# A third pair of query buffers, other places for some work of ScalarE and VectorE, and an end flag made and read earlier, in a fused attention and mixture-of-experts kernel

## The chip, the core and the metric

The kernel runs on one core of a Trainium2 chip. The metric is device time in microseconds, from start to end of one launch; lower is better. The kernel before was run three times: 861.81, 862.79 and 864.39 us, median 862.79 us.

## The reference, cut to what matters

Attention with a squared ReLU instead of a softmax, for 8 batches of 3072 rows, and then a mixture of 8 experts with one expert for each token and room for 768 tokens in each expert:

```python
scores = scale * np.matmul(z, z.transpose(0, 2, 1))     # z: 8 x 3072 x 64
attn = np.maximum(scores, 0.0) ** 2
x = (u * np.matmul(attn, v)).reshape(B * S, D)          # u, v: 8 x 3072 x 256
expert_idx = np.argmax(x @ w_gate, axis=1)              # 8 experts, capacity 768
for i in range(N):                                      # in order of the tokens
    e = expert_idx[i]
    if counts[e] < capacity:
        disp[e, counts[e]] = x[i]; counts[e] += 1       # kept, in the next free row
h = np.maximum(np.einsum('ecd,edf->ecf', disp, w1), 0.0)
y = np.einsum('ecf,efd->ecd', h, w2)
out[i] = gate_w[i] * y[expert_idx[i], pos[i]]           # only for kept tokens
```

Once all eight experts are full, no later token has an effect, so the attention of later rows need not be computed.

## The kernel before

**Stages.** The attention runs in groups n of 384 query rows (3 tiles of 128), 8 groups for each batch. With these inputs it runs groups 0 to 17 whole and the first part of group 18; then a flag says that every expert is full. The experts follow (from 605.87 us on in the profile), 16 blocks of 384 rows, each through w1 and w2.

**A group.** A group has 12 doubles c = 0 to 11, each of two chunks of 128 keys. TensorE (PE) makes scores in bursts of four doubles (`burst`, `scores`, the matmuls of L725): at c = 0 the scores of doubles 3 to 6, at c = 4 those of 7 to 10, at c = 8 those of double 11 and of doubles 0 to 2 of the next group. ScalarE (ACT) does the ReLU (`do_relu`, L533) and the square (`do_square`, L537) of each double, VectorE (DVE) splits the result into a high and a low half (`do_hi`, L1052, `do_lo`, L1058), and PE weighs v with it (`weigh`, 18 matmuls for a double, L760 to L764). ACT runs three doubles ahead of PE: in its step c it squares double c + 3 and relus double c + 4. A burst waits until the scores before it have been read (`relu_done`). Values go in high and low halves through three matmuls each, to keep precision.

**Queries and keys.** The group loop is a runtime loop, so the queries of a group are copied to fixed buffers, in two copies with the halves of partitions exchanged: `q_now` for the scores of the group itself and `q_next` for the first three doubles of the next group. GpSimd (POOL) issues these copies in `queries`, at the end of its body for group n, behind the three indirect DMAs that scatter the rows of group n - 1 to the experts (L446), the reading of the flag, the wait for these scatters to land (`scattered`, after which it frees the row buffer, `row_free`) and the wait for the burst at c = 8. PE waits for `loaded_q_now` at c = 0.

**The rows of the group before.** While PE weighs group n, the other engines route the rows of group n - 1. DVE takes them out of PSUM (`gate_x`, L1101 and L1105, at the end of its step c = 11 of group n - 1), ACT takes sums of their absolute values (L559) and high halves (L564), DVE the low halves (L1199), SyncE's queue (SP) transposes them with three DMAs (L303, `xT`), and PE multiplies with `w_gate` (L842, logits) inside double 3, behind a wait for `loaded_xT`. DVE finds each row's expert (`route_rows`, at its c = 3), PE counts (`counts_of_tiles`, L781 and L784, behind the burst at c = 4), and DVE makes positions, slots and the flag `full` (L1152 to L1172). PE's matmuls of double 4, tile 2, wait for `counts_read`.

**The flag.** `both_parts` gives each engine's body two parts with `load_end` between them: wait for `flag_ready`, load `full` into the register that ends the loop, skip the second part if it is zero. With `END_AT` = 5, PE, ACT, SP and POOL read it with double 5 done, DVE one step before. At the end, PE waits for the drains of ACT (L639) and DVE (L1357), `attention_over`, before its first matmul of the experts.

**Work for the next batch and the experts** has fixed places in the steps. In groups 1, 2, 9, 10 and 17 ACT takes four sums of |v| (`v_sum`, L508), one in each of its steps 6, 7, 8 and 9 (`SUM_AT`), each followed by a wait for its own semaphore. In groups 3 and 11 the norms of z are taken and DVE makes new scales in its steps 8 to 10. In group 8 ACT makes the high halves of the first expert's weights (`split_w_hi`, L636) in steps 7, 8 and 10, and DVE takes the maxima of the second expert's weights (`w_max`, L1323) in groups 8 to 11 (`W_MAX1_IN`). At the start of groups 0, 8 and 16 SP loads the next batch's z and v (L317, L322).

**Group 0** is written out by hand (`peeled`). In it the last quarter of the keys is made by ACT with two copies (`z_hi`, L520) in its step 1, behind the ReLU of double 5, and by DVE (L1010, L1017). PE needs those keys, and the ReLU of double 6, for its burst at c = 4.

## Time and profile before

| | kernel before |
|---|---|
| three runs, median | 861.81, 862.79, 864.39; 862.79 us |
| the profiled execution | 863.23 us, of which the span from the first to the last instruction is 861.4 us |
| PE busy with matmuls | 834.5 us (97% of the span) |
| PE weight loads (beside the matmuls) | 667.3 us (77%) |
| DVE busy | 630.0 us (73%) |
| ACT busy | 567.0 us (66%) |
| POOL busy | 170.4 us (20%) |
| mean granted TensorE clock | 0.996 |

Read it so: the span is the part that the instructions fill, and 1.8 us of the profiled execution lie around it. A PE that is busy 97% of the span leaves 26.9 us in which it does nothing, and a time at half clock counts as busy. The list of waits says what PE waited for; the chain of work that ended last, in order of time, gives the starts of PE's bursts, from which a group's length can be read; the timelines of ACT and DVE show how far ahead of PE they are.

### The profile page before, as it was taken

The numbers are of one execution on the slowest core, as the hardware profiler recorded it, in microseconds if no ns is written. First come the engines' busy times: TensorE is split into PE (matmuls) and PEld (weight loads), VectorE is DVE, ScalarE is ACT, GpSimd is POOL, SyncE is SP. The second block draws the span as 40 slices with busy tenths as digits, with TensorE's granted clock in tenths as the row PEclk, the third lists the DMA queues.
The fourth block names the chain that finished last, engine by engine and source line by source line (L and its number), as shares of the span: only waits on it lengthen the run. The fifth ranks groups of instructions, "written<-read, shape, count | busy, mean of one in ns | idle before, by whom it ended". The sixth has DMA issues, their size and how long they took to land.

```text
span 861.4 us, 25760 instructions
## 1 busy us (share of the span) xinstructions
PE 834.5 (97%) x8414; PEld 667.3 (77%) x8414; DVE 630.0 (73%) x1354; ACT 567.0 (66%) x866; POOL 170.4 (20%) x204
## 2 busy tenths in 40 slices
PE   6899999999999979999999999999999999999997
PEld 5778778788888868778788888887777777777776
DVE  7886877889989858887888888777554655565521
ACT  7877776778877758776878787678534434435422
POOL 3002112112221203202302311210121221211212
PEclk9999999999999989999999999999999999999999
DMA  7923244264334733233324425722616325415101
GB/s 290 377 80 113 55 156 179 59 187 166 118 86 128 264 88 110 84 99 110 120 78 131 139 60 156 284 61 73 156 44 167 115 68 159 143 46 152 55 18 37
DMA packets 109399, 107.90 MB, mean 125 GB/s; under 512 B 68749, under 2 KB 95578, under 8 KB 108352
## 3 DMA queue, kind: packets, MB, share of 16 engines
q1 hardware_dynamic: 100640, 87.29, 33.0%
q0 software_dynamic: 8736, 20.31, 6.7%
q8 instruction: 14, 0.23, 0.1%
q14 instruction: 9, 0.07, 0.0%
HBM read 40.03 MB, written 44.93 MB: 99 GB/s over the span
## 4 chain that ended last, share of the span: by engine, by line
PE 72%; issue 6%; DVE 6%; ACT 6%; DMA 5%; SPq 3%; DVEq 1%; ACTq 1%; POOL 0%; POOLq 0%
PE Sc L893 15%; PE O L760 11%; PE Sc L725 11%; PE O L764 10%; PE O L762 10%; PE O L916 3%; PE O L918 3%; PE O L920 3%; DMA xT<-xrow 2%; SPq L303 2%; DVE attn_hi L1052 2%; PE Sc L918 2%; PE Sc L916 2%; PE Sc L920 2%; ACT attn L533 2%
## 5 line engine op out<-in xcount | busy, mean ns | idle before, releaser
L760 PE MATMUL O<-vS,attn_hi 128*128 128x256 f16 x1332 | 363.4, 273 | 1.7 <-DVE vS L1036 1.7
L762 PE MATMUL O<-vS,attn_hi 128*128 128x256 f16 x1332 | 363.1, 273 | 0.0
L764 PE MATMUL O<-vS,attn_lo 128*128 128x256 f16 x1332 | 363.0, 273 | 0.0
L533 ACT ACTIVATE attn<-Sc 128x768 f32<-128x768 f32 x226 | 179.6, 795 | 61.5 <-PE Sc L725 58.3
L1058 DVE TENSOR_TENSOR attn_lo<-attn,attn_hi 128x768 f16<-128x768 f32 x224 | 214.4, 957 | 6.5
L537 ACT ACTIVATE attn<-attn 128x768 f32<-128x768 f32 x225 | 189.5, 842 | 10.1 <-ACT xT L508 2.9
L1052 DVE CAST attn_hi<-attn 128x768 f16<-128x768 f32 x224 | 125.0, 558 | 58.2 <-ACT attn L537 48.1
L760 PEld LDWEIGHTS O<-vS,attn_hi 128*128 128x128 f16 x1332 | 130.1, 98 | 29.3 <-issue 11.7
L764 PEld LDWEIGHTS O<-vS,attn_lo 128*128 128x128 f16 x1332 | 130.3, 98 | 15.2
L762 PEld LDWEIGHTS O<-vS,attn_hi 128*128 128x128 f16 x1332 | 130.3, 98 | 14.2
L1368 DVE SCALAR_TENSOR_TENSOR rawv<-Sc,rawv 128x768 f16<-128x768 f32 x63 | 60.2, 956 | 110.5 <-ACT rawv L646 61.2
L446 POOL DMA_INDIRECT disp<-xrow,slot x54 | 64.6, 1196 | 361.3 <-DVE slot L1171 350.4
L646 ACT ACTIVATE rawv<-Sc 128x768 f16<-128x768 f32 x63 | 51.0, 810 | 100.9 <-PE Sc L893 99.7
L725 PE MATMUL Sc<-q_now,zP 64*128 64x128 f16 (+1 forms) x801 | 90.4, 263 | 5.2 <-DMA q_now<-zQ 4.6
L725 PE MATMUL Sc<-q_now,zQ 64*128 64x128 f16 (+1 forms) x801 | 89.9, 263 | 0.0
L893 PE MATMUL Sc<-vS,w1h 128*128 128x384 f16 x384 | 78.1, 326 | 0.0
L725 PEld LDWEIGHTS Sc<-q_now,zP 64*128 64x128 f16 x801 | 55.3, 95 | 25.6 <-issue 16.1
L916 PE MATMUL O<-w2s,rawv 128*128 128x256 f16 x256 | 69.8, 273 | 0.0
L920 PE MATMUL O<-w2s,rawv 128*128 128x256 f16 x256 | 69.8, 273 | 0.0
L918 PE MATMUL O<-w2s,rawv 128*128 128x256 f16 x256 | 69.8, 273 | 0.0
L485 POOL DMA_INDIRECT out<-attn,vS x48 | 47.0, 979 | 114.0 <-ACT attn L658 100.8
L725 PEld LDWEIGHTS Sc<-q_now,zQ 64*128 64x128 f16 x801 | 55.1, 95 | 6.9
(167 smaller groups left out, 1025.0 us busy)
## 6 DMA issues: line engine op xcount, KB each, us to landing
out<-empty SPq DMA_DIRECT2D x16, 1536.0 KB, 5.9
wraw<-in_moe_w SPq DMA_DIRECT2D x16, 1024.0 KB
rawv<-in_v SPq DMA_DIRECT2D x14, 768.0 KB, 7.9
ubuf<-in_u SPq DMA_DIRECT2D x19, 384.0 KB, 3.2
disp<-vS SPq DMA_DIRECT2D x8, 774.0 KB, 11.5
rawz<-in_z SPq DMA_DIRECT2D x3, 768.0 KB
q_now<-zP POOLq DMA_DIRECT2D x18, 96.0 KB, 4.2
q_now<-zQ POOLq DMA_DIRECT2D x18, 96.0 KB, 4.2
```

The costliest lines, as they stand in the source:

```text
L533: act.activation(attn_place(c), score_place(c), ACT.Relu).then_inc(s["relu_done"], 1)
L537: act.activation(attn[:, c % BUFS, :, :], attn[:, c % BUFS, :, :], ACT.Square, scale=ROOT_C).then_inc(s["square_done"], 1)
L725: ins = nc.tensor.matmul(to, keys[r], queries[r][:, columns], start=at == 0, stop=at == len(terms) - 1)
L760: nc.tensor.matmul(o_part(t), hi, v[:, 0:D], start=c == 0 and j == 0 and t % 2 == 0, stop=False, skip_group_check=True)
L762: nc.tensor.matmul(o_part(t), hi, v[:, D:2 * D], start=False, stop=False, skip_group_check=True)
L764: ins = nc.tensor.matmul(o_part(t), lo, v[:, 0:D], start=False, stop=c == PAIRS - 1 and j == 1, skip_group_check=True)
L893: ins = nc.tensor.matmul(Sp[:, 2 * (p % 2) + fi, 0:GROUP], w[par][:, m, f * P:(f + 1) * P], xt[k][:, x + m, :], start=(at == 0), stop=(at ...
L916: nc.tensor.matmul(y_part(t), hi, w2s[:, par, f, 0:D], start=f == 0, stop=False, skip_group_check=True)
L918: nc.tensor.matmul(y_part(t), hi, w2s[:, par, f, D:2 * D], start=False, stop=False, skip_group_check=True)
L920: ins = nc.tensor.matmul(y_part(t), lo, w2s[:, par, f, 0:D], start=False, stop=f == FC - 1, skip_group_check=True)
L1052: dve.tensor_copy(attn_hi[:, b, :, :].rearrange("p j n -> p (j n)"), attn[:, b, :, :].rearrange("p j n -> p (j n)")).then_inc(s["hi_done"], 1)
L1058: dve.tensor_tensor(attn_lo[:, b, :, :], attn[:, b, :, :], attn_hi[:, b, :, :], ALU.subtract).then_inc(s["lo_done"], 1)
```

## The change

- A third pair of query buffers, `q_last`. Double 11's scores take their queries from it and no longer from `q_now`, so `q_now` is free after the burst at c = 4. POOL issues the copy to `q_now` for the next group as the first thing of its second part, after a wait for that burst and ahead of the wait for `scattered` and of `row_free`. The copies to `q_last` and `q_next` are issued where those to `q_now` and `q_next` were; PE waits for `q_last` at c = 8.
- ACT's four sums of |v| stand together in its step 7 (`SUMS_AT`), and so do the four conversions of the first expert's weights in group 8 (`W_HI_IN`). DVE's four maxima of the second expert's weights are all in its step 8.
- In group 0, ACT's two copies for the last keys go to steps 0 and 1, ahead of the ReLU of double 3 and of the square of double 4; DVE's part of them goes ahead of its v conversion. The scaling of `w_gate` goes from DVE's steps 8 and 10 to steps 5 and 7.
- The flag: DVE keeps, from step to step, how many rows each expert still lacks (`need`, times 1024, and zero when no group follows). When the counts arrive, one instruction subtracts them (`lack`) and a maximum over the experts, with a zero beside them, is the flag. Before, the flag took a sum, a subtraction, a minimum and a comparison, between steps of the routing. `END_AT` is 4: the flag is read with double 4 done (DVE: with its step 3 done), and if it is zero the group ends there. The test itself is the same: it goes on while an expert lacks rows.

The diff, without declarations of buffers:

```diff
             queries(q_now, 1, "loaded_q_now")
+            queries(q_last, 1, "loaded_q_last")
             queries(q_next, 2, "loaded_q_next")
...
                 def rest():
+                    wait_apart(pool, s["scores_ready"], n * PAIRS + PAIRS - 1)
+                    queries(q_now, n + 1, "loaded_q_now")
                     wait_apart(pool, s["scattered"], n * 48)
                     pool.sem_inc(s["row_free"], 1)
...
                     wait_apart(pool, s["scores_ready"], n * PAIRS + PAIRS + BURST - 1)
-                    queries(q_now, n + 1, "loaded_q_now")
+                    queries(q_last, n + 1, "loaded_q_last")
                     queries(q_next, n + 2, "loaded_q_next")
...
                         if peeled and c in V0_AT:
                             v_hi(UNIT * (2 + V0_AT.index(c)), UNIT * (2 + V0_AT.index(c)))
+                        if peeled and c in LAST_KEYS_AT:
+                            z_hi(3 * SLICE * P, 1, c == LAST_KEYS_AT[1], SLICE * P)
                         if c % BURST == 0:
                             do_relu(K0 + c + 3, c + 3)
                         do_square(K0 + c + 3, c + 3)
                         if c % BURST != BURST - 1:
                             do_relu(K0 + c + 4, c + 4)
-                        if peeled and c == LAST_KEYS_AT:
-                            z_hi(3 * SLICE * P, 1, False, SLICE * P)
-                            z_hi(3 * SLICE * P, 1, True, SLICE * P)
...
-                    if c in SUM_AT:
+                    if c == SUMS_AT:
                         def sums():
-                            q = (g & 2) * 2 + SUM_AT.index(c)
                             wait_apart(act, s["loaded_zv"], (n & 120) * 10 + 80)
                             act.wait_ge(s["logits_ready"], n)
-                            v_sum(q, q * UNIT, UNIT).then_inc(s["vsum_done"], 1)
-                            wait_apart(act, s["vsum_done"], (n & 120) + (g & 2) * 2 + SUM_AT.index(c) + 1)
+                            for q in range(UNITS // 2):
+                                at = (g & 2) * 2 + q
+                                v_sum(at, at * UNIT, UNIT).then_inc(s["vsum_done"], 1)
+                                wait_apart(act, s["vsum_done"], (n & 120) + at + 1)
...
-                            ins = scores(n, c, par)
+                            ins = scores(n, c, par, q_last if c == PAIRS - 1 else q_now)
                         else:
-                            ins = scores(n + 1, c - PAIRS, 0 if peeled else None)
+                            ins = scores(n + 1, c - PAIRS, 0 if peeled else None, q_next)
...
                             if not peeled:
+                                wait_apart(pe, s["loaded_q_last"], n * 32)
                                 wait_apart(pe, s["loaded_q_next"], n * 32)
...
+                    dve.scalar_tensor_tensor(out=lack[0:1, 0:E], in0=small_counts[0:1, TILES * E:(TILES + 1) * E],
+                                             scalar=-MANY, in1=need[0:1, :], op0=ALU.mult, op1=ALU.add)
                     dve.tensor_tensor(base[:, 1, :], base[:, 0, :], small_counts[:, TILES * E:(TILES + 1) * E], ALU.add)
                     dve.tensor_tensor(posf[:, :, :], counts, over_tiles(base[:, 0, :]), ALU.add
                                       ).then_inc(s["counts_read"], 1)
                     dve.wait_ge(s["counts_read"], n)
-                    dve.tensor_tensor(over[:, :], base[:, 1, :], limit[:, :], ALU.subtract)
+                    dve.tensor_reduce(full[0:1, 0:1], lack[0:1, :], AX.X, ALU.max).then_inc(s["flag_ready"], 1)
+                    dve.tensor_scalar(going[:, :], xrow[0:1, 0, D + 1:D + 2].bitcast(I32), float((NG - 2) * GROUP), MANY,
+                                      ALU.is_lt, ALU.mult)
                     route(dve.tensor_tensor(fullp[:, :, :], posf[:, :, :], over_tiles(limit[:, :]), ALU.is_ge))
-                    dve.tensor_reduce(least[:, :], over[:, :], AX.X, ALU.min)
+                    dve.tensor_tensor(need[:, :], limit[0:1, :], base[0:1, 1, :], ALU.subtract)
                     route(dve.scalar_tensor_tensor(out=posf[:, :, :], in0=fullp[:, :, :], scalar=float(FAR // 2),
                                                    in1=posf[:, :, :], op0=ALU.mult, op1=ALU.add))
-                    dve.tensor_scalar(full[0:1, 0:1], least[0:1, :],
-                                      0.0, float(NG + 1), ALU.is_lt, ALU.mult
-                                      ).then_inc(s["flag_ready"], 1)
+                    dve.tensor_scalar(need[:, :], need[:, :], going[:, 0:1], None, ALU.mult)
...
-SUM_AT = (6, 7, 8, 9)
+SUMS_AT = 7
 W_MAX0_AT = 6
-W_MAX1_IN = ((8, 8), (9, 9), (10, 9), (11, 6))
-W_HI_IN = ((8, 7), (8, 8), (8, 10), (9, 10))
+W_MAX1_IN = ((8, 8), (9, 8), (10, 8), (11, 8))
+W_HI_IN = ((8, 7), (8, 7), (8, 7), (8, 7))
...
-FIRST_ACT = (6, 7, 8, 9, 10)
+FIRST_ACT = (6, 7)
...
-END_AT = 5
-GATE_AT = (8, 10)
+END_AT = 4
+GATE_AT = (5, 7)
...
-LAST_KEYS_AT = 1
+LAST_KEYS_AT = (0, 1)
```

## Rows read from the trace of the kernel before

**Rows 1.** Waits of PE: line, what for; us in total, times, longest.
```profile
PE O L842 <- DMA xT<-xrow: 6.9, 9, 1.4
PE Sc L725 <- DMA q_now<-zQ: 4.6, 1, 4.6
PE Sc L725 <- ACT attn L533: 2.3, 1, 2.3
```

**Rows 2.** Chain that ended last, in order of time: start us, length us, what.
```profile
282.04 2.07 PE Sc L725 x36
...
290.18 6.53 DMA disp<-xrow,slot
299.28 6.54 DMA q_now<-zQ
...
306.78 4.03 PE Sc L725 x36
319.22 2.07 PE Sc L725 x36
...
350.70 2.07 PE Sc L725 x36
...
475.45 2.07 PE Sc L725 x36
485.59 2.07 PE Sc L725 x36
495.63 2.07 PE Sc L725 x36
505.96 2.07 PE Sc L725 x36
```

**Rows 3.** Stretches: bounds, length, PE, PEld, DVE, ACT, POOL busy; clock, DMA share, GB/s.
```profile
307.00:312.00 5.00, 5.00 (x47) 3.17 (x43) 0.00 (x0) 1.02 (x2) 0.00 (x0) 0.59 0.55 94
```

**Rows 4.** DMA issues from 0 to 66 us: KB each, median us to landing.
```profile
q_next<-zQ POOLq DMA_DIRECT2D x1, 96.0 KB, 8.4
```

**Rows 5.** ACT's timeline in group 2, steps 6 to 8.
```profile
103.41 0.83 ACT L508 ACTIVATE xT<-rawv 128x768 f16 x1
...
104.61 0.84 ACT L537 ACTIVATE attn<-attn 128x768 f32<-128x768 f32 x1 [0.27 <-issue]
...
108.12 0.81 ACT L533 ACTIVATE attn<-Sc 128x768 f32<-128x768 f32 x1 [1.74 <-PE Sc L725]
```

**Rows 6.** DVE's timeline in group 3, the first split behind the burst at c = 8.
```profile
141.94 0.56 DVE L1052 CAST attn_hi<-attn 128x768 f16<-128x768 f32 x1 [3.04 <-ACT attn L537]
```

**Rows 7.** PE's timeline in group 18, the logits.
```profile
597.91 0.44 PE L842 MATMUL O<-wgs,xT 128*128 128x16 f16 x12 [0.64 <-DMA xT<-xrow]
```

**Rows 8.** ACT's timeline in group 8, the first conversion of weights.
```profile
291.18 1.15 ACT L636 ACTIVATE w1h<-wraw,wscale 128x1024 f16<-128x1024 f32 x1 [0.52 <-DVE wscale L1346]
```

**Rows 9.** ACT's timeline in group 0: step 0, and the keys in step 1.
```profile
23.86 0.81 ACT L533 ACTIVATE attn<-Sc 128x768 f32<-128x768 f32 x1 [1.28 <-PE Sc L725]
...
28.52 0.93 ACT L520 ACTIVATE zQ<-rawz,zscale 64x768 f16<-64x768 f32 x1
29.48 0.93 ACT L520 ACTIVATE zP<-rawz,zscale 64x768 f16<-64x768 f32 x1
```

**Rows 10.** DVE's timeline in group 8: counts taken up, and the flag.
```profile
284.33 0.16 DVE L1152 TENSOR_TENSOR base<-base,O 128x8 f32<-128x8 f32 x1
...
285.20 0.14 DVE L1161 TENSOR_SCALAR full<-least 1x1 int32<-1x1 f32 x1
```

**Rows 11.** DVE's timeline in group 18: its last two splits.
```profile
603.10 0.95 DVE L1058 TENSOR_TENSOR attn_lo<-attn,attn_hi 128x768 f16<-128x768 f32 x1
...
604.55 0.96 DVE L1058 TENSOR_TENSOR attn_lo<-attn,attn_hi 128x768 f16<-128x768 f32 x1
```

**Rows 12.** Chain that ended last, at the end of the attention.
```profile
604.66 0.31 DVEq L258
...
605.62 0.23 PE O L732
```

More of the change, by code:

```diff
@@ L36 @@
 NORMS_FROM = 80
+MANY = 1024.0
 RING = 4
@@ L79, in relu2_attention_moe @@
         q_now = [sb(f"q_now{k}", [P, GROUP], F16) for k in range(2)]
+        q_last = [sb(f"q_last{k}", [P, GROUP], F16) for k in range(2)]
         q_next = [sb(f"q_next{k}", [P, GROUP], F16) for k in range(2)]
@@ L115, in relu2_attention_moe @@
         wg = sb("wg", [P, DC, E], F32)
-        top = sb("top", [P, TILES], F32)
+        tops = sb("tops", [P, 2 * TILES], F32)
+        top, kmax = tops[:, 0:TILES], tops[:, TILES:2 * TILES]
         below = sb("below", [P, TILES, E], F32)
@@ L120, in relu2_attention_moe @@
         key = sb("key", [P, TILES, E], F32)
-        kmax = sb("kmax", [P, TILES], F32)
         onehot = sb("onehot", [P, TILES + 1, E], F16)
@@ L124, in relu2_attention_moe @@
         limit = sb("limit", [P, E], F32)
-        over = sb("over", [P, E], F32)
+        lacks = sb("lacks", [1, 2 * E + 2], F32)
+        need, lack, going = lacks[:, 0:E], lacks[:, E:2 * E + 1], lacks[:, 2 * E + 1:2 * E + 2]
         posf = sb("posf", [P, TILES, E], F32)
@@ L129, in relu2_attention_moe @@
         row = sb("row", [P, 1], F32)
-        least = sb("least", [P, 1], F32)
-        full = sb("full", [1, 1], I32)
+        full = sb("full", [1, 1], U32)
         dues = sb("dues", [1, RING], I32)
@@ L223, in relu2_attention_moe @@
             y_scattered3 fac_ready h_first hh_first due_ready loaded_early
-            loaded_q_now loaded_q_next loaded_k_next weighed counts_read"""
+            loaded_q_now loaded_q_last loaded_q_next loaded_k_next weighed counts_read"""
         s = {n: sem(n) for n in names.split()}
@@ L700, in wait_keys, with scores @@
                         pe.wait_ge(s[key], value * 8)
-            def scores(n, c, par):
+            def scores(n, c, par, copied):
                 def key_cols(z16, k_first, r):
@@ L707, in key_cols, with query_cols @@
                     return k_first[half(r), c * P:(c + 1) * P] if par is None else z16[half(r), par * S + at:par * S + at + P]
-                def query_cols(z16, q_first, q_rest, r):
+                def query_cols(z16, q, r):
                     if isinstance(n, int):
                         return z16[half(r), n * GROUP:(n + 1) * GROUP]
-                    return (q_first if par is None else q_rest)[half(r), :]
+                    return q[half(r), :]
                 high_keys, low_keys = (
@@ L716, in scores @@
                 high_queries, low_queries = (
-                    [query_cols((zP, zQ)[x], q_next[x], q_now[x], r) for x, r in ((h, 0), (1 - h, 1))] for h in range(2))
+                    [query_cols((zP, zQ)[x], copied[x], r) for x, r in ((h, 0), (1 - h, 1))] for h in range(2))
                 terms = ((high_keys, high_queries), (high_keys, low_queries), (low_keys, high_queries))
@@ L741, in _ @@
             for c in range(BURST - 1):
-                ins = scores(0, c, 0)
+                ins = scores(0, c, 0, q_next)
             ins.then_inc(s["scores_ready"], BURST - 1)
@@ L972, in _ @@
             dve.memset(onehot[:, TILES, :], 0.0)
+            dve.memset(need[:, :], capacity * MANY)
+            dve.memset(lack[:, E:E + 1], 0.0)
             def bits(exponent):
@@ L1202, in part @@
                                 ins.then_inc(s["rows_lo"], 1)
-                        if peeled and c in V0_AT:
-                            first_v(2 + V0_AT.index(c))
                         if not peeled and (c == ZLO_AT or c in VLO_AT):
@@ L1219, in part @@
                                         only_if(dve, n == 4 + q, lambda: w_max(0, 0, q))
-                        if peeled and c == LAST_KEYS_AT:
+                        if peeled and c == LAST_KEYS_AT[1]:
                             dve.wait_ge(s["zhi_ready"], 8)
@@ L1224, in part @@
                             z_lo_across(3 * SLICE * P, 1)
+                        if peeled and c in V0_AT:
+                            first_v(2 + V0_AT.index(c))
                         if not peeled and c == ROUTE_AT:
```

## The prediction

> **What bounds the kernel now.** I read three views in this order. First the page: PE is busy for 834.5 of 861.4 us, so only 26.9 us of idle time, the time at half clock, and matmuls that are left out can be won; no saving on DVE, ACT or POOL counts by itself. Then the list of PE's waits [rows 1]: a wait for the queries, once, 4.6 us; nine waits for the transposed rows `xT`, 6.9 us in all; and one for ACT's ReLU, 2.3 us. Last the chain in order of time, whose pieces "PE Sc L725 x36" are the bursts [rows 2]. In an undisturbed group they stand at c = 4 (475.45), c = 8 (485.59), c = 0 of the next group (495.63) and c = 4 again (505.96): 10.14 + 10.04 + 10.33 = 30.51 us for a group. A burst takes 2.07 us, so a double takes (10.04 - 2.07) / 4 = 1.99 us. What a group takes above 30.51 us is what the change can win in it.
>
> **The queries of group 9.** From c = 4 of group 8 (282.04) to c = 4 of group 9 (319.22) it is 37.18 us, 6.67 more than 30.51 [rows 2]. The wait at c = 0 is 4.6 of it [rows 1]; in the rest PE works at a lower granted clock: 0.59 on average from 307 to 312 us, so mostly at 1.2 instead of 2.4 GHz [rows 3], and the burst behind the wait takes 4.03 instead of 2.07 us [rows 2]. The cause is an order on POOL: the last scatter was issued at 290.18 and landed 6.53 us later, since the next batch's v was being loaded; only behind it POOL went on to the copies, the second of which was issued at 299.28 and landed 6.54 us later, at 305.82, 3.6 us behind the place where c = 0 would have been (292.18 + 10.04 = 302.2) [rows 2]. With the change the copies are issued right behind the third scatter, whose issue ends at about 291.2; the burst that they now wait for ended at 284.1. Two copies of about 0.6 us each, so the second starts by about 292.5. The longest landing of a 96 KB copy under full DMA load is 8.4 us [rows 4]; with it the queries are there at 300.9, 1.3 us ahead of 302.2. With the 6.54 us of the row before it is 3.2 us. What else is queued behind the moved copies on POOL: the wait for `scattered` and `row_free`, which DVE needs only at about 301.6; and two more copies in each group behind the burst at c = 8, about 1.2 us on an engine that is busy 20% of the span. No idle time at PE, so no reason for the clock to fall. I take the whole **6.7 us**. DMA speaks against it most: the Trainium skill, "DMA: Bandwidth & Descriptors", section "Issuing engines are not separate DMA queues", says that DMAs of all engines run on the same 16 DMA engines and interleave; so a copy that is started earlier is started into the batch load. That is what the 8.4 us is taken from (it landed amid such a load), and by it the margin is 1.3 instead of 3.2 us, not gone.
>
> **The sums of |v|.** Groups 2, 3, 10 and 11 take 0.9 to 1.0 us more than 30.51 from burst to burst; group 10's row stands: 350.70 - 319.22 = 31.48 [rows 2]; the sum over the four is 3.8 us. Group 18 has the same wait, 0.64 us of idle time, about 0.8 with the refilling [rows 7]. All five follow a group with sums, and the plain groups 5, 6, 7 and 13 to 17 have no such wait. A sum takes 103.41 to 104.61 = 1.2 us of ACT with the wait for its own semaphore [rows 5]. Two of the four lie ahead of the burst at c = 8, where ACT then still idles 1.74 us [rows 5]; the two behind it delay the squares of doubles 12 and 13, DVE's splits, `gate_x`, and the transposes by 2.1 to 2.4 us, of which 0.95 reach PE. So the chain has 1.1 to 1.4 us of slack. With all four in step 7 the pause ahead of the ReLU of double 11 is 1.74 + 2 x 1.2 = 4.1 us, and four sums take 4 x 1.2 = 4.8, or 5.3 if the address arithmetic between sums, now not hidden by other work, adds 0.1 each: ACT comes 0.7 to 1.3 us late, against 1.1 to 1.4 us of slack. What is left at PE is 0 to 0.2 us for each group; I take 0.1. Gain: 3.8 + 0.8 - 5 x 0.1 = **4.1 us**, between 0 (if a sum in a row of sums took 1.5 us or more) and 4.6.
>
> **Weights in group 8 and the maxima.** Four conversions of 1.15 us from 291.18 on [rows 8] end at 295.6; the burst's ReLU could start at 292.18 + 2.07 + 0.1 = 294.4. ACT is 1.2 us late, inside the same slack: 0, at worst 0.2. DVE's maxima move by at most two steps; the one that comes to step 8 of group 11 falls into a pause like that of group 3, where DVE idles for 3.04 us [rows 6]: 0. The excess of groups 4 and 12 (1.1 us each, from DVE's scales in steps 9 and 10), of group 8 (0.5) and group 1 (1.5, of which a slow third transpose is most) stays.
>
> **Group 0.** PE waits 2.3 us at its burst at c = 4 for the ReLU of double 6 [rows 1]. Ahead of it ACT makes the two key copies, 0.96 us apart [rows 9]. One of them goes in front of the ReLU of double 3, where ACT idles for 1.28 us [rows 9]: hidden. The other stays ahead of double 6's ReLU. DVE then has the keys ready earlier and is not late for double 4. Gain **0.95 us**; the bounds are 0.9 and, if both hid, 1.9. The scaling of `w_gate` moves in DVE's slack: 0.
>
> **The flag.** (a) At the end, one double is left out in group 18. PE would win 1.99 us, but what ends the attention is DVE's drain: its last split starts at 604.55 and PE's first matmul behind it is at 605.62 [rows 11, 12]. DVE's last split becomes that of double 6, at 603.10, 1.45 us earlier [rows 11]; the two instructions more in front of it cost 0.08 each. Gain 1.45 - 0.16 = **1.3 us**. (b) In every group PE now reads the flag one double earlier. The flag was written at 285.20 + 0.14 = 285.34, 3.3 us behind the burst's start at 282.04 [rows 2, 10]; made of two steps it comes about 0.4 us sooner. Double 4 ends at 282.04 + 2.07 + 0.2 (counts) + 1.99 = 286.3, so 1.0 us, or 1.4 with the shorter chain, lie between. Reading it and branching took DVE's sequencer about 0.96 us from the start of the load to the drain's end [rows 11, 12]. If PE's sequencer is that fast and ahead of its array, it has branched at 286.3 or before. Before, the same read stood behind double 5 and nothing shows: 10.14 us between c = 4 and c = 8, with the counts in it, against 10.04 without [rows 2]. So PE's sequencer hides the read; cost 0, bounds 0 and 0.3 us for each of 18 groups. Queued behind the wait is double 5, which only PE's own next burst and DVE's reuse of the buffers wait for. The Trainium skill, "Advanced Engine Details and Errata", section "Engine Queue Depths", gives TensorE's queue 64 instructions on trn2. By it the sequencer stands far ahead and would reach the flag before it is written, so that the flag's own time decides: 285.0 + 0.96 = 286.0, still ahead of 286.3. (c) On DVE the same two small instructions in 18 groups lie in its pauses: 0.
>
> **The sum.** 6.7 + 4.1 + 0.95 + 1.3 = 13.0 us. The experts' stage is bound by PE and is not touched. Profiled execution: 863.2 - 13.0 = 850.2 us; it lies 0.4 above the median of the runs shown, so I expect a median of **850.0 us**.
>
> **Rivals.**
> 1. The sums don't fit: a sum behind a sum needs 1.5 us or more, ACT is 2 us late or more, and the transposes wait as before. For it: each sum waits for its own semaphore and nothing fills the gap; the pause is short by 0.7 us even by my count. Against it: 1.2 us is measured with that wait. Gain 8.9 us: 854; in between, 851.5 to 854.
> 2. PE's read of the flag shows in part, 0.1 to 0.3 us a group, 2 to 5 us: 852 to 855.
> 3. The copies still come late in group 9, or another wait there takes their place (the transposes of group 9, whose wait is hidden today behind that for the queries): at worst all 6.7 us stay, 856.7.
> 4. The change doesn't do what it says at the end: group 18 stops no earlier, or a wait for first rows takes the place of the drain: 1.3 us less, 851.3. It is inside the range of the forecast.
> 5. Slower: PE's sequencer is not ahead at double 4, because it has just waited there for `counts_read`. Then the array idles for the read and the branch, 0.96 us in each of 18 groups [rows 11, 12], 17.3 us: 850.0 + 17.3 = 867.3. It ends above the time before once a group loses more than 13.0 / 18 = 0.72 us. Against it stands the hidden read behind double 5, which also has no long queue in front of it.
> 6. More than computed: both key copies hide, the first transposes of group 1 come on time: up to 2.5 us more, 847.5.
>
> **Chances.** Forecast as worked out, 848.8 to 851.4: 0.55. Sums partly or not hidden: 0.17. Flag in part: 0.09. Copies or transposes in group 9: 0.05. More than computed: 0.08. Slower by the flag: 0.03. Nothing that can be measured, by several of these together: 0.03. Some 0.3% (2.6 us) is what a measurement of this kernel can tell from no change. Range 847.0 to 856.0 us, which holds all but the last two cases and the worst of rival 3. Faster by over 0.3%: 0.94; within: 0.03; slower: 0.03.
>
> **What the profile after would show.** No wait of PE for `q_now` and no stretch under full clock between 300 and 320 us; c = 4 to c = 4 of 30.5 us into groups 2, 3, 9, 10, 11 and 18, with the list of waits naming `xT` in groups 1, 4, 8 and 12 alone, some 4 us in all; the burst at c = 4 of group 0 at 31.2 instead of 32.1; six matmuls less in each of L760, L762 and L764 (one double); PE's first matmul of the experts about 13 us earlier, at 593. If the interval from c = 4 to c = 8 grows above 10.14 us in all groups, the flag is read too early. If ACT's ReLU of double 11 starts more than 1.4 us behind the burst's end in groups 1, 2, 9, 10 and 17, the sums are too long for their pause.

## The result and the profile after

The changed kernel takes 852.08 us (median of 852.00, 852.02, 852.14 and 852.44); the kernel before, on the same chip, 863.44 us (median of four, 861.81 to 864.39). The ratio is 0.9871, with a 95% interval of 0.9854 to 0.9888. I forecast 850.0 us, in a range of 847.0 to 856.0; the time lies in the range, but above the 848.8 to 851.4 us of the forecast as worked out. The profiled execution after takes 852.0 us, its span 850.2 us, against 863.2 and 861.4 before.

The waits of PE in the kernel after (line, what for; us in total, times, longest) stand beside [rows 1]:

```profile
PE O L848 <- DMA xT<-xrow: 4.8, 8, 0.8
PE O L737 <- DVE ones L973: 4.5, 1, 4.5
PE O L765 <- DVE vS L1044: 1.6, 1, 1.6
PE Sc L730 <- ACT attn L538: 1.5, 1, 1.5
PE O L737 <- DVEq L1367: 0.7, 1, 0.7
```

The wait for `q_now` is gone. The one for `xT` has fallen from 6.9 to 4.8 us, and it still comes eight times, in groups 2, 3, 4, 8, 10, 11, 12 and 18: I expected four, in groups 1, 4, 8 and 12. The second and third row are in the start of the kernel, as before.

The chain of the kernel after, in order of time, its bursts: c = 4 of group 8, c = 8, c = 0 of group 9, c = 4 of groups 9 and 10, and then four bursts of an undisturbed stretch (c = 8 of group 14, and c = 0, 4 and 8 of group 15).

```profile
279.65 2.07 PE Sc L730 x36
...
289.79 2.07 PE Sc L730 x36
...
299.82 2.07 PE Sc L730 x36
...
310.16 2.09 PE Sc L730 x36
...
341.35 2.09 PE Sc L730 x36
...
475.92 2.07 PE Sc L730 x36
485.96 2.07 PE Sc L730 x36
496.30 2.07 PE Sc L730 x36
506.44 2.07 PE Sc L730 x36
```

Into group 9 it takes 310.16 - 279.65 = 30.51 us, the undisturbed length, where it took 37.18 [rows 2]. Into group 10 it takes 31.19 us, where it took 31.48 and where I expected 30.6. From c = 4 to c = 8 it is still 506.44 - 496.30 = 10.14 us. A stretch of the table by windows (bounds, length, PE, PEld, DVE, ACT, POOL busy; clock, DMA share, GB/s) shows the full granted clock, 1.00, where [rows 3] had 0.59:

```profile
307.00:312.00 5.00, 5.00 (x75) 3.91 (x72) 4.26 (x14) 2.91 (x5) 0.00 (x0) 1.00 0.37 105
```

Burst by burst, the first matmuls of the bursts in both traces give the places where the 11.2 us of span went:

| place | before | after | gained |
|---|---|---|---|
| start and group 0, up to c = 0 of group 1 | 52.31 | 51.68 | 0.63 |
| group 1, c = 0 to c = 4 | 11.88 | 10.34 | 1.54 |
| groups 2, 3, 10, 11: what they take over 30.51 from c = 4 to c = 4; group 18: over 10.34 from c = 0 to c = 4 | 4.57 | 3.61 | 0.96 |
| group 9, c = 8 to c = 4 | 27.04 | 20.38 | 6.66 |
| groups 4 and 12 together; 7 and 8 together | | | 0.21; -0.14 |
| c = 4 of group 18 to the first matmul of the experts | 6.92 | 5.62 | 1.30 |
| the experts | 255.5 | 255.5 | 0.0 |

The gains add to 11.16 us. (An interval starts with the first matmul of its burst, which in the chain is up to 0.1 us later.) The burst at c = 4 of group 0 starts at 31.48 where I expected 31.2, and the first matmul of the experts at 594.68 where I expected 593.

### The profile page after: what moved, and what is told of

It reads as the page before. It is cut to its first block, busy times and chain, and to the rows that moved or that the text cites. A ratio compares the mean times of both kernels' runs of the same rounds, so it can differ in the third digit from the quotient of the medians.

```text
span 850.2 us, 25682 instructions
## 1 busy us (share of the span) xinstructions
PE 831.2 (98%) x8396; PEld 665.1 (78%) x8396; DVE 631.2 (74%) x1390; ACT 567.6 (67%) x864; POOL 191.5 (23%) x240
## 4 chain that ended last, share of the span: by engine, by line
PE 67%; issue 10%; ACT 8%; DVE 6%; DMA 3%; SPq 2%; DVEq 1%; ACTq 1%; POOL 0%; POOLq 0%
PE Sc L899 15%; PE O L765 10%; PE Sc L730 9%; PE O L767 9%; PE O L769 9%; ACT attn L538 4%; PE O L922 3%; PE O L926 3%; PE O L924 3%; DVE attn_hi L1060 2%; SPq L305 2%; DMA xT<-xrow 2%; PE Sc L922 2%; PE Sc L926 2%; PE Sc L924 2%
## 5 line engine op out<-in xcount | busy, mean ns | idle before, releaser
L730 PE MATMUL Sc<-q_now,zP 64*128 64x128 f16 (+1 forms) x648 | 77.0, 270 | 0.7 <-issue 0.6
L730 PE MATMUL Sc<-q_now,zQ 64*128 64x128 f16 (+1 forms) x648 | 76.7, 270 | 0.0
L730 PEld LDWEIGHTS Sc<-q_now,zP 64*128 64x128 f16 x648 | 45.8, 94 | 17.5 <-issue 8.3
L899 PEld LDWEIGHTS Sc<-vS,w1h 128*128 128x128 f16 x384 | 37.6, 98 | 21.0
```

Source lines behind the costliest of these rows:

```text
L730: ins = nc.tensor.matmul(to, keys[r], queries[r][:, columns], start=at == 0, stop=at == len(terms) - 1)
L899: ins = nc.tensor.matmul(Sp[:, 2 * (p % 2) + fi, 0:GROUP], w[par][:, m, f * P:(f + 1) * P], xt[k][:, x + m, :], start=(at == 0), stop=(at ...
```

## Experiments

All twelve kernels also cut the value that SP waits for before it loads the first early rows, in the last groups, to its low 16 bits; the first of them is the changed kernel with nothing but that. "Kernel before" is always the one on the same chip.

**1. The changed kernel again.**

```diff
-                        sp.reg_load(due, dues[0:1, bass.ds((n - 1) & (RING - 1), 1)])
+                        sp.reg_load(due_raw, dues[0:1, bass.ds((n - 1) & (RING - 1), 1)])
+                        sp.reg_mov(due, sp.snap(due_raw) & 65535)
```

> The changed kernel as it is, with one register operation more on SyncE's queue (a mask on a value that it loads, from group 16 on). Both theories: 852.1 us, and per group the same lengths as in the profile of the changed kernel: 30.5 us for a plain group, and 0.6 to 0.9 us more into each of the five groups behind ScalarE's sums.

852.04 us (851.82 to 853.68), ratio 0.9873 [0.9848, 0.9898]: the mask costs nothing, and this is the base for the others.

**2. The sums in their old places.**

```diff
-SUMS_AT = 7
+SUM_AT = (6, 7, 8, 9)
...
-W_MAX1_IN = ((8, 8), (9, 8), (10, 8), (11, 8))
-W_HI_IN = ((8, 7), (8, 7), (8, 7), (8, 7))
+W_MAX1_IN = ((8, 8), (9, 9), (10, 9), (11, 6))
+W_HI_IN = ((8, 7), (8, 8), (8, 10), (9, 10))
```

> The changed kernel with the sums of |v|, the conversions of the first expert's weights and the maxima back in their old steps. Theory of the prediction (four sums in the pause are nearly hidden, worth 4.1 us): 856.2 us. Theory from the profile after (ScalarE still comes 1.9 us late instead of 2.1 us, so the sums' move is worth 0.8 us in five groups; the conversions' move keeps some 0.9 us out of group 9, which has no wait for the rows now): 853.8 us, with a wait for the transposed rows in group 9.

853.41 us (853.11 to 854.74), ratio 0.9882 [0.9859, 0.9905]: 1.4 us more than with the sums together, not 4. In its trace groups 2, 3, 10, 11 and 18 have all of their 0.8 to 1.0 us again (4.6 us). So the regrouping is worth about 1 us. The wait for `xT` in group 9 that I expected from the conversions in their old steps is not there: that group takes 30.51 us here too, so moving the conversions gained nothing that this trace shows. What in the changed kernel undoes it stands in ACT's timeline in group 2 (start us, us, instruction, idle before and its end), the counterpart of [rows 5]:

```profile
101.32 0.84 ACT L542 ACTIVATE attn<-attn 128x768 f32<-128x768 f32 x1
102.18 0.84 ACT L513 ACTIVATE xT<-rawv 128x768 f16 x1
...
103.41 0.84 ACT L513 ACTIVATE xT<-rawv 128x768 f16 x1 [0.29 <-ACT xT L513]
...
104.62 0.84 ACT L513 ACTIVATE xT<-rawv 128x768 f16 x1 [0.28 <-ACT xT L513]
...
105.84 0.84 ACT L513 ACTIVATE xT<-rawv 128x768 f16 x1 [0.28 <-ACT xT L513]
106.59 0.18 ACT L513 ACTIVATION_READ_ACCUMULATOR xT<-rawv  x1
107.78 0.81 ACT L538 ACTIVATE attn<-Sc 128x768 f32<-128x768 f32 x1 [1.00 <-ACT xT L513]
```

The sums (named `xT<-rawv` here) are 1.21 to 1.23 us apart, as I had computed. But between the end of the last, 106.77, and the ReLU of double 11 lies 1.0 us in which ACT does nothing. A sum's own wait explains 0.28 of it. Most of the rest could be the four branches of the weights' conversions, which the change has put into the same step in four separate conditions and which are passed over in this group. The burst at c = 8 started at 103.61; in groups without sums the ReLU follows 2.29 us behind such a start. Here it comes 4.17 us behind: 1.88 us late.

**3. One branch in place of four.**

```diff
-                    for q, (group, at) in enumerate(W_HI_IN):
-                        if c == at:
-                            only_if(act, n == group, lambda: split_w_hi(0, 0, q))
+                    if c == SUMS_AT:
+                        def conversions():
+                            for q in range(4):
+                                split_w_hi(0, 0, q)
+                        only_if(act, n == 8, conversions)
```

> The changed kernel, with one branch instead of four around the four conversions of group 8's weights, all of which stand behind the sums in ScalarE's program in step 7. In the trace of the changed kernel the last sum of group 2 ends at 106.77 us and the ReLU of double 11 starts at 107.78; four branches of about 0.15 us lie between. If the lateness is sums plus branches, ScalarE is 3 x 0.15 = 0.45 us less late (1.4 instead of 1.9 us), the waits for the transposed rows in groups 2, 3, 10, 11 and 18 shrink from about 0.7 to about 0.24 us each, and the time falls by some 2.2 us to 849.9. If the branches are hidden beside other work and the sums' length alone counts, the ReLU starts where it did and the time stays at 852.1.

850.48 us (849.76 to 852.21), ratio 0.9857 [0.9841, 0.9872]. The same place of ACT's timeline in group 2 of this kernel:

```profile
106.13 0.84 ACT L515 ACTIVATE xT<-rawv 128x768 f16 x1 [0.28 <-ACT xT L515]
106.88 0.18 ACT L515 ACTIVATION_READ_ACCUMULATOR xT<-rawv  x1
107.61 0.81 ACT L540 ACTIVATE attn<-Sc 128x768 f32<-128x768 f32 x1 [0.55 <-ACT xT L515]
```

The idle time is 0.55 instead of 1.00 us: 0.15 for each branch taken away. The ReLU is 1.43 us late, and groups 3, 10 and 11 take 0.23 to 0.25 us above the undisturbed length instead of 0.67 to 0.72. The branches were on the path. The five groups gain 2.3 us; group 1 gives 0.99 of it back, of which more in experiments 11 and 12.

**4. Two wide sums in place of four, and one branch.** The edit of experiment 3 and this one:

```diff
-                            for q in range(UNITS // 2):
-                                at = (g & 2) * 2 + q
-                                v_sum(at, at * UNIT, UNIT).then_inc(s["vsum_done"], 1)
-                                wait_apart(act, s["vsum_done"], (n & 120) + at + 1)
+                            for q in range(2):
+                                at = (g & 2) + q
+                                v_sum(at, at * (2 * UNIT), 2 * UNIT, spare).then_inc(s["vsum_done"], 2)
+                                wait_apart(act, s["vsum_done"], (n & 120) + at * 2 + 2)
```

> The changed kernel with two sums over six chunks in place of four over three, and with one branch in place of four ahead of the four conversions of weights in ScalarE's step 7. Theory from the profile after (ScalarE's ReLU of double 11 is 1.88 us late, of which the sums take 4.9 us where the pause is 3.8, and four branches of 0.15 us stand behind them; up to 1.2 us late costs nothing): two sums save about 1.0 us, three branches 0.45 us, so it is 0.4 to 0.5 us late and the wait for the rows is gone in the five groups: 852.1 - 3.6 = 848.5 us. Rival (the wait for the rows comes from something other than ScalarE's lateness, such as VectorE or the transposes): 851.5 to 852.1 us.

848.91 us (848.16 to 849.81), ratio 0.9828 [0.9804, 0.9852]. The ReLU is 0.10 us late, and none of the five groups waits for `xT`.

**5. Two wide sums, the four branches left.** The edit of experiment 4 without that of experiment 3.

> The changed kernel with two sums over six chunks of v in place of four over three, and the four branches left as they are. With one branch the wide sums left the ReLU of double 11 only 0.10 us late, and three branches more cost 0.45 us, as measured with the narrow sums. So it is about 0.55 us late, less than the 1.2 us that the chain has, and no wait for the transposed rows is left in groups 2, 3, 10, 11 and 18: 3.6 us less than the changed kernel. TensorE's program is laid out as in the changed kernel, so its load should start at 62.4 us and group 1 take 10.34 us: 852.1 - 3.6 = 848.5 us, or somewhat less if part of group 3's wait is larger than computed. Rival: the sums are not what the chain waits for; then the time stays above 851.

848.82 us (848.15 to 850.57), ratio 0.9836 [0.9816, 0.9855]. The waits of PE, and ACT's timeline in group 2:

```profile
PE O L739 <- DVE ones L975: 4.5, 1, 4.5
PE O L850 <- DMA xT<-xrow: 2.0, 3, 0.8
```

```profile
102.77 1.48 ACT L515 ACTIVATE xT<-rawv 128x1536 f16 x1 [0.29 <-ACT xT L515]
104.16 0.19 ACT L515 ACTIVATION_READ_ACCUMULATOR xT<-rawv  x1
105.26 0.81 ACT L540 ACTIVATE attn<-Sc 128x768 f32<-128x768 f32 x1 [0.91 <-PE Sc L732]
```

A sum over twice the chunks takes 1.48 instead of 2 x 0.84 us and saves one read of the accumulator and one wait. The ReLU is 0.57 us late here. The three waits left are those of groups 4, 8 and 12. The changed kernel and experiments 3, 5 and 4 make a series, read in groups 9 and 10: late by 1.89, 1.44, 0.57 and 0.10 us in group 9, group 10 takes 0.67, 0.23, 0 and 0 us more. In experiment 7, where the ReLU is 1.06 us late, group 10 has no wait for `xT` either. So the chain behind the ReLU has about 1.2 us of slack, and between 1.44 and 1.89 us late, 0.45 us more of lateness cost 0.44 us. This kernel and that of experiment 4 are some 3.2 us faster than the changed one, the best of these, and not told apart.

**6. The copies to `q_now` behind the landing of the scatters again.** The third pair of buffers stays.

```diff
-                    wait_apart(pool, s["scores_ready"], n * PAIRS + PAIRS - 1)
-                    queries(q_now, n + 1, "loaded_q_now")
...
                     wait_apart(pool, s["scores_ready"], n * PAIRS + PAIRS + BURST - 1)
+                    queries(q_now, n + 1, "loaded_q_now")
```

> The changed kernel with three pairs of query buffers, but with the copy to q_now issued where it was, behind the scatters and the burst at c = 8. Theory (the order on GpSimd cost the 4.6 us of waiting and the low clock behind it): 852.1 + 6.7 = 858.8 us, with a wait for q_now in group 9 of about 4.6 us and a granted clock well below full behind it, and nothing in other groups. Rival (the third buffer alone, or something else of the change, took the wait away): 852 us.

859.36 us as median of seven (855.55 to 860.40), ratio 0.9944 [0.9926, 0.9962]: 7.3 us more than in experiment 1. The profiled execution is the fastest of the seven and shows another loss in its place: its list of waits has no `q_now`, but a longest wait for `xT` of 2.1 us, in group 8, where the third transpose took 4.2 us. Behind that wait the granted clock fell: the burst at c = 4 took 3.39 instead of 2.07 us (a row of the chain, and one of the table by windows).

```profile
PE O L849 <- DMA xT<-xrow: 6.5, 8, 2.1
```

```profile
281.81 3.39 PE Sc L731 x36
```

```profile
281.00:285.00 4.00, 4.00 (x41) 2.31 (x39) 1.64 (x8) 0.22 (x1) 0.00 (x0) 0.57 0.90 301
```

With group 8 held up, the copies, issued from 297.1 on and landed 4.3 to 4.7 us later, by 302.1, were there before the burst at c = 0 was due (303.3). So this trace doesn't show the mechanism that the experiment was made for. The median agrees with the 6.7 us, and the order on POOL is the only thing that differs from experiment 1; how the 7.3 us are divided no trace of a slower execution shows. The wait itself stands in the traces of two kernels with the old order, the kernel before (4.6 us) and that of experiment 10 (4.7 us).

**7. The flag written last.** The maximum that makes the flag goes from behind `posf` to the end of the routing.

```diff
-                    dve.tensor_reduce(full[0:1, 0:1], lack[0:1, :], AX.X, ALU.max).then_inc(s["flag_ready"], 1)
...
                     dve.tensor_copy(base[:, 0, :], base[:, 1, :])
+                    dve.tensor_reduce(full[0:1, 0:1], lack[0:1, :], AX.X, ALU.max).then_inc(s["flag_ready"], 1)
```

> The changed kernel, with the flag's last instruction (the maximum over the lacking counts) moved to the end of the routing, behind the copy of the running counts. The flag is then written about 4.3 us behind the start of the burst at c = 4 instead of 2.7, while double 4 ends at 4.27. Theory: TensorE's sequencer reads the flag and branches in about 0.96 us while the array works, and has 1.5 us to do it in the changed kernel; here nothing is left of that, so from c = 4 to c = 8 it takes 10.14 + about 1.0 us in each of 18 groups, about 18 us in all: 870. Rival: the read needs less than the 0.96 us that were seen on VectorE (0.3 to 0.5): 5 to 9 us more, 857 to 861. If the wait is free even here (the sequencer is not what holds the array), the time stays at 852.

868.71 us (868.07 to 869.95), ratio 1.0072 [1.0058, 1.0086]: slower than the kernel before. In the chain of this kernel, c = 4 and c = 8 of group 15 are 11.25 us apart instead of 10.14; its list of waits has 17 new ones, which the profile puts down to the split that ended last, and one more in group 18:

```profile
508.46 2.07 PE Sc L732 x36
...
512.72 0.05 DVE full L1184
...
519.71 2.07 PE Sc L732 x36
```

```profile
PE O L767 <- DVE attn_lo L1068: 16.4, 17, 1.2
...
PE O L858 <- DVE full L1184: 1.0, 1, 1.0
```

The flag's users, in the view by tile (line, engine, operation, times: durations in ns, start in us), in group 15 of the changed kernel and of this one:

```profile
L1166 DVE TENSOR_REDUCE full<-lacks x1: 149/149/149, 498.9 to 498.9; 1x1 uint32<-1x9 f32 x1
L260 PEldq TENSOR_LOAD <-full x1: 301/301/301, 499.3 to 499.3; - x1
```

```profile
L1184 DVE TENSOR_REDUCE full<-lacks x1: 142/142/142, 512.6 to 512.6; 1x1 uint32<-1x9 f32 x1
...
L260 PEldq TENSOR_LOAD <-full x1: 302/302/302, 513.0 to 513.0; - x1
```

In both PE's sequencer stands at the flag and loads it 0.34 us behind the start of DVE's instruction. The first matmul behind double 4 is due 4.16 us behind the first matmul of the burst (508.39), at 512.54. It comes 1.1 us later, at 513.64 in PE's timeline, 1.01 us behind the start of DVE's instruction (512.63):

```profile
512.63 0.14 DVE L1184 TENSOR_REDUCE full<-lacks 1x1 uint32<-1x9 f32 x1
```

```profile
512.43 0.27 PE L771 MATMUL O<-vS,attn_lo 128*128 128x256 f16 x1
513.64 0.28 PE L767 MATMUL O<-vS,attn_hi 128*128 128x256 f16 x1 [0.94 <-DVE attn_lo L1068]
```

In the other groups it is 1.01 to 1.05 us too (1.22 in group 1). In the changed kernel the same 1.0 us end at 498.95 + 1.0 = 499.95, and the matmul is due at 500.39. The read is hidden with 0.4 us to spare. Eighteen reads of 1.1 us are 20 us; 16.7 are seen, since the pause in every group also gives the sums the time they lack (the waits for `xT` fall from 4.8 to 1.6 us).

**8. The old flag, read behind double 4.** The four steps of the kernel before, with `END_AT` = 4.

```diff
+                    dve.tensor_tensor(over[:, :], base[:, 1, :], limit[:, :], ALU.subtract)
...
+                    dve.tensor_reduce(least[:, :], over[:, :], AX.X, ALU.min)
...
+                    dve.tensor_scalar(full[0:1, 0:1], least[0:1, :],
+                                      0.0, float(NG + 1), ALU.is_lt, ALU.mult
+                                      ).then_inc(s["flag_ready"], 1)
```

> The changed kernel, with the flag made in the old way (four steps, written 3.4 us behind the start of the burst at c = 4 instead of 2.7), but read behind double 4 all the same. Double 4 ends at 4.27, so 0.9 us are left for a read of about 0.96. If that is the length of the read on TensorE's sequencer, 0 to 0.1 us shows in a group: 852 to 854. Rival: the sequencer needs the 1.4 us that the new flag leaves, and each of 18 groups takes 0.3 to 0.5 us more, 857 to 861: then the faster flag is a condition of the early read. Group 18 ends as in the changed kernel.

853.36 us (852.98 to 855.18), ratio 0.9895 [0.9878, 0.9912]. Its chain in group 15:

```profile
496.83 2.07 PE Sc L732 x36
507.12 2.07 PE Sc L732 x36
```

Here c = 4 and c = 8 are 10.29 us apart; the flag's last step starts at 500.00. So 0.15 us show in this group, 0.12 to 0.2 in most: 2.6 us by this reading, of which some comes back in the waits for `xT` (3.6 instead of 4.8 us). The flag's start stands 2.65, 3.17 and 4.17 us behind the burst in the three kernels; 0, 0.15 and 1.11 us show. The early read needs the shorter flag, but only for about 0.15 us a group; in the medians, taken on two chips, it is 1.3 us in all.

**9. The exit behind double 5.**

```diff
-END_AT = 4
+END_AT = 5
```

> The changed kernel, with the exit behind double 5 of the last group instead of double 4; the flag is still made in two steps. If the gain at the end is DVE's last split standing 1.3 us earlier, this takes 1.3 us more, 853.4, and the stretch from the burst at c = 4 of group 18 to the experts' first matmul grows from 5.6 to 6.9 us. If the read of the flag behind double 4 costs anything in a group, part of it comes back here: every 0.05 us a group would be 0.9 us, and the time would be 852.5 or less.

854.09 us (853.64 to 855.28), ratio 0.9901 [0.9885, 0.9917]. From c = 4 of group 18 to the first matmul of the experts it takes 7.08 us, against 5.62: the exit one double earlier is worth 1.46 us. PE waits 0.2 us for DVE's drain instead of 0.7. No interval from c = 4 to c = 8 is shorter than in the changed kernel, so the read behind double 4 costs nothing.

**10. The last keys alone.** The kernel before with the new places of the two key copies in group 0 and, in the same group, DVE's part of those keys ahead of its v conversion. The scaling of `w_gate` stays where it was.

```diff
+                        if peeled and c in LAST_KEYS_AT:
+                            z_hi(3 * SLICE * P, 1, c == LAST_KEYS_AT[1], SLICE * P)
...
-                        if peeled and c == LAST_KEYS_AT:
-                            z_hi(3 * SLICE * P, 1, False, SLICE * P)
-                            z_hi(3 * SLICE * P, 1, True, SLICE * P)
```

> The kernel before with one part of the change alone: in group 0 the first of ScalarE's two key copies stands ahead of the ReLU of double 3, and VectorE scales w_gate behind the keys. From the burst at c = 1 to that at c = 4 it took 10.44 us before and 9.63 in the changed kernel. If the move does it by itself, it is 9.6 here too and the time is 0.8 us less than before, 862.6; if the changed kernel's gain came from something else as well (another start, the queries' copies), it stays at 10.0 or more and less than 0.4 us is gained. Group 1's slow third transpose, 4.1 us, should stay as in the kernel before, since nothing in TensorE's program moves; were it gone, the move of the keys would be what cured it.

861.29 us (860.27 to 863.22), before 863.25: ratio 0.9982 [0.9970, 0.9995]. From c = 1 to c = 4 it is 9.63 us, as in the changed kernel, and PE's wait for ACT 1.5 us instead of 2.3. The other 1.2 us between the medians are not explained by the move. In the profiled execution group 1 came without its excess, against what I expected. The move of the keys is not its cure: experiments 2, 3, 4 and 11 have it too, and a slow transpose in group 1.

**11 and 12. The place of PE's instructions.** I had not forecast that group 1 would lose its 1.54 us. The view by tile says of the three transposes of that group in the kernel before, and of those in the kernel after:

```profile
DMA to landing us min/median/max: 2.4/2.5/4.1
```

```profile
DMA to landing us min/median/max: 2.4/2.4/2.5
```

And the DMA view of the stretch in which the last two are under way (58.0 to 61.5 us in both) has this row in the kernel before only:

```profile
q8 instruction: 1, 0.02, 2.1%
```

It is a load of 16 KB of instructions. I asked whether the place of PE's instructions in its program sets when it comes: the kernel of experiment 4, where it also fell among the transposes, with six instructions more ahead of group 0, and the changed kernel with six less.

```diff
-            turn_over(90)
+            turn_over(93)
```

> The kernel with two wide sums and one branch (848.9 us, group 1 from burst c = 0 to c = 4 in 12.0 us, its third transpose landing in 4.4 us while a 16 KB instruction load that started at 59.8 us was under way), with three warm-up matmuls more ahead of group 0 (93 instead of 90). Nothing else changes than that all of TensorE's later instructions lie six places further back in its program, exactly where they lie in the changed kernel, whose load started at 62.4 us, behind the transposes. Theory: the place of TensorE's instructions in the program sets when the load starts, and the load delays a transpose that is under way. Then the load starts at about 62.3 here, the third transpose lands in 2.4 us, group 1 takes 10.3 us, and the time is 848.9 - 1.5 = 847.4 us. Rival: the load follows ScalarE's program or chance; the time stays at 848.9 us or differs from run to run.

```diff
-            turn_over(90)
+            turn_over(87)
```

> The changed kernel with three warm-up matmuls less (87 instead of 90), so that TensorE's instructions lie six places further forward, where they lie in the two kernels with one branch. By the theory that the place in the program starts the load: the load starts at 59 to 60 us, the third transpose of group 1 lands in some 4 us, group 1 takes 11.3 to 12.0 us between its bursts instead of 10.34, and the time is 852.1 + 1.0 to 1.5 = 853.3 us. If the load has another cause, the time stays at 852.1 us.

Both expectations failed. The first took 849.72 us (849.06 to 851.71; ratio 0.9847 [0.9827, 0.9867]), with the load still among the transposes; the second 852.21 us (851.84 to 854.03; ratio 0.9880 [0.9860, 0.9901]), with the load still behind them. Rows of the first, the view by tile in group 1 and the DMA view from 57.5 to 61 us:

```profile
DMA to landing us min/median/max: 2.5/3.5/4.4
```

```profile
q8 instruction: 1, 0.02, 2.5%
```

So the six places do not decide it. Nor do PE's own instructions: experiment 10 has the same ones as the kernel before, and its load came at 62.6 instead of 60.8 us. What goes together in all fourteen profiled executions is the load and the slow transpose. In five (the kernel before, experiments 2, 3, 4 and 11) the load started at 58.5 to 60.8 us, and a transpose took 3.7 to 4.4 us; group 1 then lost 0.8 to 1.7 us. In nine it started at 61.9 us or later, and all three took 2.5 us or less. Experiment 6 shows the pair a sixth time, in group 8. In the fourteen executions there are 756 such transposes. Seven took 3.5 us or more, all in these six groups, and in no other group did a 16 KB load start among the transposes. That the load is the cause is the likely reading, not shown: no experiment moved the load at will. The four executions of experiment 4 had spans of 846.3, 846.5, 847.7 and 848.0 us, and the profiled one, with the slow transpose, was the last: this looks like something that differs from execution to execution of one kernel.

## Why the prediction was right or wrong

The range held and the sign was right. The sum of 13.0 us missed one term by 3.1 us, which is rival 1's case (851.5 to 854 us), and an effect outside the sum gave back 1.5, which is part of rival 6. That the profiled execution came so near to the sum is in this part luck.

- **Queries, 6.7: 6.66 in the traces.** The copies were issued at 288.90 and 289.46, right behind the third scatter's issue, and landed after 3.9 and 5.1 us, well under the 8.4 taken as the worst. I had expected the later of them by 292.5 in the time of the trace before, in which this group stands 2.4 us later: 290.1 here. The Trainium skill's page "DMA: Bandwidth & Descriptors", "Issuing engines are not separate DMA queues", spoke for a copy slowed by the batch load. The trace agrees: the DMA share was 0.89 from 288 to 293 us, and the same copies landed after 1.9 to 2.2 us in most other groups. The margin was 5 us all the same. Rival 3 did not come.
- **Sums, 4.1: 0.96 in the traces. The step that failed** is the lateness of ACT. I put it at 0.7 to 1.3 us against a slack of 1.1 to 1.4; the slack is 1.2 and was right, the lateness is 1.88. Two things were missing, and they explain most of it. The pause from the last square's end (102.16) to the place where the ReLU would have started (103.61 + 2.29 = 105.90) is 3.7, not 4.1 us. And behind the sums I counted no branches: the change puts four conditional conversions into the same step, and skipping them costs 0.15 us each in every group. Experiment 3 takes 0.45 us of it away, experiment 5 the length of the sums, and each removes the part of the wait that the slack predicts. It is rival 1 by its effect, but not by its mechanism: a sum in a row of sums needs 1.21 to 1.23 us, not 1.5.
- **Weights in group 8, 0 to 0.2:** in group 9 there is no wait for `xT`; the ReLU was 1.1 us late, inside the slack. Right. The two instructions more on DVE were costed at 0 in the groups; group 8 takes 0.12 us more than before, and whether they are the reason was not tested.
- **Keys, 0.95: 0.80**, and by themselves, as experiment 10 shows. The kernel after started its first bursts 0.2 us later, which no term held; the traces don't say why.
- **The end, 1.3: 1.30.** What PE waits for ahead of the experts is DVE's drain (0.7 us), as forecast. Experiment 9 puts the exit's own worth at 1.46 us, where I had 1.45; with the late exit that stretch takes 0.16 us more than in the kernel before, which is what I had put down for the two instructions more on DVE.
- **The flag's read, 0: 0.** The interval stayed 10.14 us. That PE's sequencer hides the read was argued from double 5 and a price of 0.96 us from DVE; experiment 7 measured 1.0 us from the start of DVE's instruction, about 0.9 from its end, and a reserve of 0.4 us. So rival 5's price was near (1.11 us in each group and 868.7 us when nothing is hidden, where 0.96 and 867.3 were written down) and its condition was false. The page "Advanced Engine Details and Errata" of the Trainium skill, "Engine Queue Depths", let PE's sequencer reach the flag before it is written; the load of the flag 0.34 us behind DVE's start, in every group, agrees with that. The lead has an end: in the kernel before, with double 5 still ahead of the flag, the load came 1.09 us behind DVE's start (286.29 against 285.20), about when the array began double 5.
- **Group 1, "stays": it went**, 1.54 us. I took a slow third transpose for a property of the kernel. It stands in the profiled execution of that kernel and not in that of experiment 10, whose program for PE is the same, while those of experiments 2, 3, 4 and 11, variants of the changed kernel, have it. So it need not belong to either kernel. The two profiled executions of the changed kernel (the result's and that of experiment 1) are without it; whether others have it is not known.

So 13.0 - 3.1 (sums) - 0.15 (keys) - 0.2 (start) + 1.5 (group 1) + 0.1 (groups 4, 7, 8 and 12) = 11.15 us.

## What to carry to other kernels

Work that is moved into a pause brings its control flow along: count the branches, address steps and waits behind it in every turn of the loop, those that are not taken too, and measure the pause from the end of the last instruction to where the next would start. A chain with slack is then a threshold: below it nothing shows, above it all does, so half a microsecond in each of five groups was worth 2 us above it (experiment 3) and nothing below it (experiments 4 and 5). And a stall that stands in one profiled execution is not yet the kernel's; before it is written into a sum as staying or going, see it in a second one.

## What the runs showed of the hardware

- A skipped branch on ACT takes 0.15 us of an otherwise idle engine (1.00 to 0.55 us for three).
- A sum on ACT over 1536 columns of fp16 takes 1.48 us, two over 768 take 2 x 0.84, and every sum brings 0.19 us for the read of the accumulator (it overlaps the sum's end by 0.1 us) and 0.28 us for the wait for it.
- From the start of the DVE instruction that writes a flag to PE's next matmul behind load and branch it takes 1.0 to 1.1 us where nothing hides it (experiments 7 and 8; 1.2 in group 1); the load itself is 0.30 us.
- One DMA transpose or two, otherwise of 2.4 us, took 3.5 to 4.4 us in each of the six cases where a 16 KB instruction load started while the three transposes of a group were under way, and none of the others, over 700, took more than 2.5 us.
- The granted clock fell at PE's wait of 4.6 us in the kernel before (0.59 on average from 307 to 312 us) and at one of 2.1 us in experiment 6 (0.57 from 281 to 285 us). The second wait cost 2.1 us by itself, and the burst behind it 1.3 us more. Behind the wait of 1.5 us in group 1 of experiment 4 the bursts kept their 2.07 us.
